# Pooled attention of a three-stage kernel: rows added in place on VectorE, keys pooled on GpSimd, weights loaded in the order of use

## What is computed

```python
factor = 4
q_d = q.reshape(B, H, Sd, factor, D).mean(axis=3)      # k_d and v_d likewise, Sd = 144
out_d = sm_attn(q_d, k_d, v_d)                         # softmax attention over 144 pooled rows
out_up = np.repeat(out_d, factor, axis=2)
mask = np.abs(pos[:, None] - pos[None, :]) < factor    # a band of seven keys for each row
...
out_local = np.matmul(attn, v)
x = (out_up + out_local)                               # -> 2304 tokens of 512
xn = x / rms * rms_g                                   # first feed-forward, 512 -> 1536 -> 512
x = (silu(xn @ w_gate) * (xn @ w_val)) @ w_out
r = np.maximum(x @ w_in, 0.0)                          # second feed-forward, 512 -> 2048 -> 512
out = (s * (r * r) + b) @ w_out2
```

## Time and profile before

| | us |
|---|---|
| median of 3 runs | 1049.47 |
| lowest and highest | 1049.28, 1050.06 |
| the profiled execution, its own time | 1050.09 |
| its span in the trace | 1048.3 |
| PE busy in the span | 965.3 |

### The profile page before, as it was taken

The page is one execution under the profiler, slowest core; times in us unless marked ns, Lnnn a source line. Parts: engine busy times, 40 slices in busy tenths (PEclk is TensorE's granted clock), DMA queues, the critical chain, the costliest instruction groups (busy, mean ns, idle before and its releaser), DMA issues.

```text
span 1048.3 us, 13187 instructions
## 1 busy us (share of the span) xinstructions
PE 965.3 (92%) x5056; PEld 783.4 (75%) x5080; DVE 557.7 (53%) x814; ACT 332.3 (32%) x722; POOL 393.4 (38%) x198
## 2 busy tenths in 40 slices
PE   3657787799899999999999999999999999999997
PEld 2545566799877767777777799887888888888896
DVE  6868966877566567556453132334443343343343
ACT  2333446222431243232324154322222232222222
POOL 3647754889387668646550055300000000000000
PEclk9999999899999999999999999999999999999999
DMA  9977443413132222201101333201100200010010
GB/s 242 261 188 190 136 128 108 122 51 118 36 116 73 66 78 91 70 10 40 64 19 42 120 115 119 69 1 41 41 1 1 80 1 1 21 41 1 1 41 21
DMA packets 54639, 77.65 MB, mean 74 GB/s; under 512 B 6224, under 2 KB 37936, under 8 KB 53680
## 3 DMA queue, kind: packets, MB, share of 16 engines
q1 hardware_dynamic: 52560, 72.09, 23.2%
q10 hardware_dynamic: 2016, 4.72, 1.2%
HBM read 66.17 MB, written 10.62 MB: 73 GB/s over the span
## 4 chain that ended last, share of the span: by engine, by line
PE 77%; DVE 7%; DMA 5%; POOL 5%; issue 4%; ACT 1%; SPq 1%; DVEq 0%; ACTq 0%; POOLq 0%
PE bank L609 25%; PE bank L717 6%; PE bank L718 6%; PE bank L719 6%; PE bank L735 6%; PE bank L736 6%; PE bank L737 6%; PE bank L632 4%; PE bank L630 4%; PE bank L631 4%; DMA rawv<-in_v_dram 3%; DVE dv L1105 2%; POOL prod L419 2%; DVE sc L439 1%; DMA ks<-in_k_dram 1%
## 5 line engine op out<-in xcount | busy, mean ns | idle before, releaser
L419 POOL TENSOR_TENSOR prod<-qs,ks 128x896 f32<-128x896 f32 x80 | 174.1, 2198 | 107.8 <-DVE sc L439 70.9
L433 POOL TENSOR_TENSOR prod<-sc,vs 128x896 f32<-128x896 f32 x80 | 150.0, 1978 | 67.2 <-DVE x L449 39.1
L756 DVE SCALAR_TENSOR_TENSOR r<-bank,r 128x512 f32<-128x512 f32 (+1 forms) x80 | 51.1, 638 | 183.8 <-ACT r L744 183.8
L719 PE MATMUL bank<-y_h,w2i_l 128*128 128x512 f32 (+1 forms) x320 | 117.7, 368 | 0.0
L651 DVE TENSOR_TENSOR bank<-bank,u 128x256 f32<-128x256 f32 (+1 forms) x72 | 40.6, 564 | 139.3 <-PE bank L609 130.8
L630 PE MATMUL bank<-h_h,wo_h 128*128 128x256 f32 (+1 forms) x288 | 107.4, 373 | 0.0
L609 PE MATMUL bank<-x_h,wv_h 128*128 128x256 f32 (+1 forms) x288 | 103.1, 374 | 1.6 <-DVE h_l L657 1.6
L744 ACT ACTIVATE r<-bank 128x512 f32<-128x512 f32 (+1 forms) x80 | 44.4, 555 | 183.8 <-PE bank L719 183.1
L609 PE MATMUL bank<-x_h,wg_h 128*128 128x256 f32 (+1 forms) x288 | 92.6, 346 | 7.0 <-ACT u L639 6.9
L632 PE MATMUL bank<-h_h,wo_l 128*128 128x256 f32 (+1 forms) x288 | 97.9, 340 | 0.0
L631 PE MATMUL bank<-h_l,wo_h 128*128 128x256 f32 (+1 forms) x288 | 97.2, 337 | 0.0
(11 more groups left out here) (118 smaller groups left out, 1966.5 us busy)
## 6 DMA issues: line engine op xcount, KB each, us to landing
raww<-in_moe_w_out_dram SPq DMA_DIRECT2D x14, 512.0 KB, 3.9
rawq<-in_q_dram SPq DMA_DIRECT2D x4, 1152.0 KB, 8.9
rawk<-in_k_dram SPq DMA_DIRECT2D x4, 1152.0 KB, 11.0
rawv<-in_v_dram SPq DMA_DIRECT2D x4, 1152.0 KB
ks<-in_k_dram SPq DMA_DIRECT2D x16, 280.0 KB
vs<-in_v_dram SPq DMA_DIRECT2D x16, 280.0 KB
raww<-in_moe_w_in_dram SPq DMA_DIRECT2D x8, 512.0 KB, 3.5
y_raw<-y_scr SPq DMA_DIRECT2D x4, 1024.0 KB, 4.8
```

The lines of the kernel that those rows point to most:

```text
L419: pool.tensor_tensor(dst, qv, kv, ALU.mult).then_inc(prod_ready, 1)
L433: pool.tensor_tensor(dst, pv, vv, ALU.mult).then_inc(prod_ready, 1)
L719: last = pe.matmul(o, w2i_l[:, m, kk, :], y_h[t % 2][:, kk, 0:w], start=False, stop=kk == DT - 1)
```

## The change

- **Pooling of q and v on DVE.** Instead of a reduction with a step of 64, two tensor_tensor additions of contiguous halves: in place in `rawq` or `rawv` (128 or 72 partitions, two row pairs at once), then into `qd` or `dv`. `pool_q` stands at heads 5 and 6 of the batch before; `pool_v` in two halves at heads 0 and 1 of its own batch (before: four quarters at heads 3 to 6 of the batch before).
- **All of k is pooled on POOL**, batch 0 too, ahead of the first product.
- **Columns of a pooled head are interleaved** by two (`v_rows`, `co` and the strided `qT` and `cs` operands of PE), so that v and the stored result move in pieces twice as long.
- **Turning.** The six units go q, k, q, k, q, k in slots 7, 8 and 9, two each, and the scores of head h wait only for the third that they need.
- **Weights.** Pieces follow the order of use in chunk 0 (`FIRST_ORDER`: gate, val, then out one pair behind). Piece 0 is loaded late in batch 2, pieces 0 and 1 are split near the end of batch 3, and the splitting of pieces 4 to 17 stands inside chunk 0, ten of them on DVE and four on POOL.
- **Tile 1.** Its `qk_reduce` is spread over steps 0 to 9 of chunk 0, `softmax_norm` moves from step 9 to 10, `add_pooled` and the root move one step later, and the four rounds of `transpose_x` stand in steps 8 to 10.
- **SP's order** is new: tile 0's rows and the raw batches alternate, weights only behind them, tile 1's loads between the pieces.

```diff
+FIRST_ORDER = [("gate", 0), ("val", 0)]
+for _j in range(1, M1 // 2):
+    FIRST_ORDER += [("gate", _j), ("val", _j), ("out", _j - 1)]
+HI_AT = {0: (4, 5), 1: (6, 7), 2: (8,), 3: (9, 10), 4: (11,), 5: (12, 13), 6: (14,), 7: (15, 16), 8: (17,)}
+LO_AT = {0: (4,), 1: (5,), 2: (7, 8), 3: (10,), 4: (11,), 5: (13,), 6: (14,), 7: (16,), 8: (17,)}
+QK1_AT = {0: (2, 3), 1: (4,), 2: (5,), 3: (6, 7), 4: (8,), 5: (9, 10), 6: (11,), 7: (12,), 8: (13,), 9: (14, 15)}
+UNIT_SLOT = {7: (0, 1), 8: (2, 3), 9: (4, 5)}
...
-                last = dve.tensor_reduce(dqk[:, n, :], rawq[:, n, :].rearrange("p t (f d) -> p t d f", f=FAC), op=ALU.add, axis=AX.X)
+                    c_link(dve.tensor_tensor(rawq[:, :, 0:2 * D], rawq[:, :, 0:2 * D], rawq[:, :, 2 * D:4 * D], ALU.add))
+                    dve.tensor_tensor(qd[:, :, :], rawq[:, :, 0:D], rawq[:, :, D:2 * D], ALU.add).then_inc(q_pooled, 1)
...
-                last = dve.tensor_reduce(dv[0:JH, b % 2, n, :], rawv[0:JH, n, :].rearrange("p t (f d) -> p t d f", f=FAC), op=ALU.add, axis=AX.X)
+                c_link(dve.tensor_tensor(rv[:, :, 0:2 * D], rv[:, :, 0:2 * D], rv[:, :, 2 * D:4 * D], ALU.add))
+                dve.tensor_tensor(dv[0:JH, b % 2, 8 * part:8 * part + 8, :], rv[:, :, 0:D], rv[:, :, D:2 * D], ALU.add).then_inc(v_pooled, 1)
...
-                    if h >= 4 and b + 1 < B:
-                        transpose_pooled(b + 1, h - 4)
+                    if b + 1 < B:
+                        for i in UNIT_SLOT.get(h, ()):
+                            turn_pooled(b + 1, i)
...
-                            last = pe.matmul(CSC[h % 2][0:JH, a * J:(a + 1) * J], qkT[0:D, b % 2, h * J + a * JH:h * J + (a + 1) * JH],
-                                             qkT[0:D, b % 2, (H + h) * J:(H + h + 1) * J], start=True, stop=True)
+                            last = pe.matmul(CSC[h % 2][0:JH, a * J:(a + 1) * J], over(qT[0:D, b % 2, h * J + a:], [[2, JH]]),
+                                             kT[0:D, b % 2, h * J:(h + 1) * J], start=True, stop=True)
...
-                if c == 0 and m < 8:
-                    qk_reduce(dve, 1, 2 * m)
...
+                    for n in LO_AT.get(m, ()):
+                        weight_lo(dve, n)
+                    for n in QK1_AT.get(m, ()):
+                        qk_reduce(dve, 1, n)
...
-                if c == 1 and m >= 8:
-                    transpose_x(pe, 2, m - 8)
+                if c == 1 and m in (9, 10):
+                    transpose_x(pe, 2, 1 if m == 9 else 3)
```

388 lines of the change are left out of this document (202 added, 186 removed).

## The result

| | before | after |
|---|---|---|
| median, us | 1049.7 | 1057.06 |
| lowest and highest of 6 runs | 1048.96, 1051.73 | 1054.99, 1059.65 |
| ratio of after to before | | 1.0067, interval 1.0051 to 1.0084 |
| profiled execution, span | 1048.3 | 1054.7 |
| first gate of chunk 0 | 164.2 | 159.7 |

The changed kernel is 7 us slower, 0.7%, and the interval of the ratio does not reach 1. The forecast was 1038 with a range to 1050, so both the time and the sign were wrong. The rest after chunk 2 is the same as before. The first 286 us gained 4.5 us up to the first gate (forecast: 13.4) and lost 10.7 behind it (forecast: 2.0).

A forecast was written before the change was run, and what follows sets the result against it. It took DMA as a second bound up to 61 us and the DVE, PE and ACT loop after. Profiled 1050.1 less 13.4 before the first gate plus 2.0 in chunks gave 1038.7, median 1038, range 1022 to 1050.

The forecast's parts named there:

- What bounds the kernel: First 286.60 us: DMA a second bound up to 61 us, the DVE, PE and ACT loop the bound after.
- POOL's k: Coarse attention: adding k on POOL, 4.2 us a batch beside 8 products of 2.1 in 33 us, is hidden.
- Start of batch 0: First `cneg` of batch 0 comes at 18.9 us instead of 22.05, with DVE's additions of q taking 2.1 us.
- Half of v: Heads 0 and 1 of each batch: two DVE additions take 2.9 us, bounds 1.88 and 4.9, against 3.86 for the reductions.
- As rival: Coarse attention: v's additions each wait for a POOL product, 4.9 us a half, kernel ends at 1055; chance 0.08.
- A batch: Coarse batches of 38.4 and 36.9 us become 32.9, including 9.3 us after head 7; bounds 31.0 and 37.0.
- Chunks 0 and 1: First gate to chunk 2: 122.4 becomes 124.4 us, step 10 unmoved relative to the gate, later `softmax_norm` chain adding 2.0.
- Weights chase chunk 0: Chunk 0: slow turns of `raww` slots put piece 17 some 12 to 14 us late, giving 1051; chance 0.12.
- Strided operands on PE: Coarse heads on PE: doubled halves of scores and transposes cost 0.8 us for 32 heads, giving 1063; chance 0.04.
- No effect: Coarse batches keep their old length under PE's loop, the start's gain of 3 is lost in the chunks: 1050; chance 0.04.
- both cheap: Halves of v at 2.2 us and low parts at 1.5 us give 1026; chance 0.22 for 1018 to 1030.
- Sum: Whole kernel: 1050.1 - 13.4 + 2.0 = 1038.7 us for the profiled execution, 1038 for the median.

The follow-up runs named there:

- e2: Changed kernel with v pooled by tensor_reduce instead of two additions, at the same place: 1054.79 us, 1.0059 of the kernel before.
- e9: Changed kernel with v's additions at heads 0 and 1 ahead of the sum that starts POOL's product: 1054.62 us, 1.0040 of the kernel before.
- e11: Kernel before with only the pooling of q and v on DVE changed, to two additions at the old places: 1063.22 us, ratio 1.0136.
- e12: e1_v_gap with raw k (and batch 1's raw q) earlier in SP's queue: 1041.61 us, 0.9919 of the kernel before.
- e13: Changed kernel with only raw k (and batch 1's raw q) earlier in SP's queue: 1055.37 us, 1.0061 of the kernel before.
- e5: Changed kernel with low parts of weight pieces 4 to 17 in chunk 0 written as zeros by memset: 1051.20 us, 1.0027 of the kernel before.
- e1_v_gap: Changed kernel with v's additions for batches 1 to 3 moved behind the last head of the batch before: 1045.84 us, 0.9960 of the kernel before.

## Why the prediction was wrong, step by step

**What bounds the kernel.** "The DVE, PE and ACT loop is the bound" past 61 us was incomplete. POOL is in the loop: its product waits for DVE's sum, DVE's next sum for the product, and behind a waiting sum stand `cneg` and the addition of q. Two steps of the prediction's coarse part fail by that: the half of a pooled v, priced by a mean over other places, and POOL's k. "The move of POOL's k (4.2 us a batch beside 8 products of 2.1)" was put down as hidden; it shows as head 7, 4.5, 3.1 and 1.0 us late in the first three batches. By POOL's busy time (19 to 27 of 34 us) there was room. But the room lies at heads 0 and 1, where POOL waits for DVE, not at head 6.

**Start of batch 0** (18.9, measured 20.53). The two additions of q took 2.11 + 2.51 us, not 2.1: they met POOL's first products and k. The forecast had used the undisturbed rows.

**Half of v** (2.9 with bounds 1.88 and 4.9, measured 3.65, and 3.99 in batch 3). This is the term with which the coarse part was mis-sized. The choice "the middle between the medians" of the earlier trace rows was wrong in kind: those low parts stand at many phases against POOL, while the additions stand right behind the sum that starts the product, so that the second one always meets it. The Trainium skill's rule ("SBUF — State Buffer", section "Who interferes with whom": a DVE instruction with two SBUF inputs contends with a GpSimd one that reads SBUF, the second waits for the end of the first, a tensor_reduce never contends) is what e2, e9 and e11 show: 2.44 us behind a product and 0.69 ahead of it, reductions at 1.91 throughout, products at 2.36 on average with additions in the kernel and 2.11 with reductions. As rival it had been given 0.08, since it asked for halves of 4.3 us; its mechanism came in every batch, at a lower price than its threshold, because the first addition mostly starts before the product and only one of the two waits.

**A batch** (32.9; measured 35.1, 35.3 and 34.1). Heads 0 and 1: 5.4 and 4.9 forecast, 6.1 and 5.6 in batch 1, 7.7 and 5.2 in batch 2 (there DVE waits another 1.6 us for a product). Heads 3 to 6 at 2.5 and 2.73 each: right, 2.61 and 2.75, only head 6 of batches 1 and 2 comes 0.5 later. Head 7 at 2.73: wrong, as above. The gap of 9.3 us: wrong in the other direction, it took 7.0, 6.5 and 6.0 us. PE turns q and k while head 7 waits, so part of what the gap was to hold was done; but in no kernel with k in time (e12, e13) was it over 8.1, so the sum of the gap was 1 us too long in any case. The last batch took 34.6 (forecast 33). The errors of the start and the four batches, 1.6 + 2.0 + 2.3 + 1.1 + 1.6, are (but for rounding) the 8.7 us by which the gate at 159.7 missed 151. In batches 1 to 3 heads 0 and 1 alone are 1.3, 2.6 and 2.0 us over, more than the 5.0 of these batches: there the late head 7 and the short gap cancel. It was luck that these two errors had opposite signs; only in batch 0, where head 6 came at 41 as forecast, does the late head 7 outweigh the gap.

**Chunks 0 and 1** (+2.0, measured +10.7). "Step 10 stays where it is relative to the gate": it came 4.6 us later. DVE's work there was forecast too dear, the low parts of w_out and w_gate have means of 1.62 and 1.79 us and not 2.11. The term that failed is the waits: 13.9 us in steps 0 to 9 where 4 to 6 were put, nearly all for ACT, which has the high parts ahead of `hidden_hi` and `silu` now. The reading of the kernel before was already short: its ten steps hold 13.5 us of DVE's waits, not 4 to 5, with DVE busy 42.4 of 55.5 us. "`softmax_norm` stands 4.5 us into step 10": right, and this move is the second loss, though it had been priced. The prediction added it to a chain that in the kernel before was not the one to set chunk 2: PE's own steps were, with the second half of tile 1 just ahead of them. Of the 2.5 us which the tail was to give back 0.8 came (28.3 us from the last sum of tile 1 to chunk 2, before 29.1), and POOL's second half of tile 1 took 2.3 us longer, 33.4 instead of 31.1: its products take the same 31.3 us in sum, but POOL waits 3.5 us for DVE's sums instead of 0.6, of which 2.3 behind `add_pooled` and a `hidden_lo` that waits for ACT's squares. 4.6 + 4.5 + 2.3 - 0.8 is the 10.7, but for 0.1.

**The other rivals.** *Weights chase chunk 0* gave 1051, and comes nearest in kind. But it named the transfers and the turns of the slots; e5 shows the subtraction and the later normalisation, and a late transfer shows once, as a wait of 2 us. *Strided operands on PE*: nothing, a head still takes 2.75 us, as forecast; the Trainium skill's statement on two accesses in a 16-byte line ("SBUF — State Buffer", section "Specifications (TRN2)") agrees. *No effect* and *both cheap* did not occur. That the stretch behind chunk 2 stays at 762 us was right.

**Sum.** 1038.7 forecast for the profiled execution, 1056.8 measured: 8.7 of the difference before the first gate, 8.7 in the chunks, 0.7 behind them and outside the span.

## What to carry to other kernels

Price an instruction where it stands, not by its mean: beside an engine that shares its reads, ask which instruction starts the other engine's work, and put the two-input one ahead of that, or where the other engine is idle. An engine that is idle a third of the time is no cover if its pauses lie elsewhere than the new work; look at which of its instructions the next engine waits for at that very place. Work taken out of a stage that has slack into one whose chain sets the end must be paid at that chain's price, and a queue that issues in order carries such a delay from one tensor to the next.

## What the hardware showed

**The clock in the coarse part.** PE's granted clock was 1.00 in all windows of the earlier trace rows up to the gate, and 0.57 to 0.60 in batches 1 to 3 after; single stretches stand at 0.50, the lower of its two levels, 1.2 GHz instead of 2.4. In e5_lo_zero, whose code is that of the changed kernel up to the first gate, one execution kept 1.00 all the way:

```profile
57.58:95.12 37.54, 26.03 (x148) 21.06 (x148) 25.45 (x34) 11.97 (x47) 20.95 (x10) 1.00 0.50 135
95.12:129.67 34.55, 26.02 (x148) 21.05 (x146) 23.86 (x27) 11.68 (x46) 25.66 (x14) 1.00 0.56 159
129.67:164.25 34.58, 22.54 (x133) 18.54 (x132) 30.73 (x41) 16.95 (x57) 19.95 (x9) 1.00 0.34 108
```

Its batches are as long as at 0.57, or longer (37.5, 34.6 and 34.6 against 35.3, 34.1 and 34.6 us), and a head takes 2.74 us at either level. With matrices of 64 to 144 columns in a loop of four engines the clock cost nothing that shows. The Trainium skill ("TensorE: Matmul & The Clock Gate", section "Terms") puts the penalty at the throttled time times one half, which for these three batches (104 us at a mean of 0.58) would be some 44 us, an estimate. Here, the longer batches at 1.00 speak against it. So do the times of the kernel before: 47 of its executions had a mean granted clock above 0.99 and 36 one of 0.92, with medians of 1049.8 and 1050.3 us.

**The clock in the chunks.** There it does cost. The timeline of PE around chunk 1's last wait in the changed kernel:

```profile
268.66 0.28 PE L659 MATMUL bank<-h_h,wo_l 128*128 128x256 f32 x1
275.31 1.12 PE L581 MATMUL bank<-ident,x 128*128 128x128 f32 x4 [6.37 <-ACT x L567]
276.07 0.56 PE L636 MATMUL bank<-x_h,wg_h 128*128 128x256 f32 x1
276.43 0.42 PE L636 MATMUL bank<-x_l,wg_h 128*128 128x256 f32 x1
```

After 6.4 us of waiting the matmuls of 256 columns run at 0.42 instead of 0.28 us, 0.22 apart instead of 0.12, until the clock is back at 1.00 at 279.9 us. The four transposes, `gate` and `val` take 5.4 us instead of the 3.3 of the next step, so this wait of PE costs some 2.1 us more than it lasts. (The whole step takes 7.7 instead of 4.7 us, but it holds one more round of transposes and a wait of 0.6 for DVE.) The changed kernel has four such slow stretches in its two chunks (around 170, 195, 230 and 275 us), the one before had one (around 200). That is 20.5 us at half clock against 6.8. Half of the difference, 6.8 us, is an estimate of the most that they could have in the 10.7 us of the chunks; no run separates them from the waits ahead of them.

**A tiny instruction can wait as long as a large one.** In e1_v_gap the tensor_scalar on 72 x 16 sums, 0.16 us elsewhere, took 2.33 us at 90.9 us, from its start to the end of the product that POOL had begun (93.2):

```profile
90.92 2.33 DVE L1161 TENSOR_SCALAR csum<-csum 72x16 f32<-72x16 f32 x1
```

The same happened at 122.3 us, and once in the kernel before (2.33 us at 101.3).
